# Turning x and z by 32x32 blocks on VectorE, scaling at the output, and turning h inside layer 2, in a kernel of windowed attention, a mixture of experts and a wide second MLP

## The reference

```python
# 1. attention: 2 x 8 heads, 768 positions, head width 64
#    scores against keys nearer than 16 positions and against 24 block summaries; softmax; values
x = attention(q, k, v).transpose(0, 2, 1, 3).reshape(1536, 512)
# 2. mixture of 8 experts, one expert for each token
logits = x @ w_gate + modality_bias[modality_id]          # 1536 x 8
e_idx = argmax(logits); gate_w = softmax(logits)[e_idx]
out[mask] = gate_w[mask, None] * (np.maximum(x[mask] @ w1[e], 0.0) @ w2[e])   # w1: 512 x 1024, w2: 1024 x 512
# 3. second MLP
h = np.maximum(out @ w_in, 0.0)                           # w_in: 512 x 2048
return (h * h) @ w_out                                    # w_out: 2048 x 512
```

## Time and profile before

| | us |
|---|---|
| median of three runs | 522.28 |
| the profiled execution | 521.77 |
| its span, first to last instruction | 520.1 |
| PE busy in the span | 508.1 |
| DVE busy | 225.4 |
| ACT busy | 188.0 |
| granted TensorE clock, mean | 0.998 |

### The profile page before, as it was taken

The page is one execution under the profiler, slowest core; times in us unless marked ns, Lnnn a source line. Parts: engine busy times, 40 slices in busy tenths (PEclk is TensorE's granted clock), DMA queues, the critical chain, the costliest instruction groups (busy, mean ns, idle before and its releaser), DMA issues.

```text
span 520.1 us, 9415 instructions
## 1 busy us (share of the span) xinstructions
PE 508.1 (98%) x3115; PEld 410.0 (79%) x3117; DVE 225.4 (43%) x440; ACT 188.0 (36%) x355; POOL 87.1 (17%) x110
## 2 busy tenths in 40 slices
PE   8889999999999999999999999999999999999995
PEld 3678788888888888888788888888888888888884
DVE  4787686974323554237632422342242233222221
ACT  1876665243524544225522212331221233122121
POOL 4434335027600223100000000300000020000002
PEclk9999999999999999999999999999999999999999
DMA  8999666384661655521200000400000020000002
GB/s 285 336 290 340 235 220 228 99 285 104 189 216 41 219 204 202 202 82 40 83 1 1 0 1 0 161 0 0 0 0 0 0 81 0 0 0 0 0 0 81
DMA packets 19018, 54.92 MB, mean 106 GB/s; under 512 B 2848, under 2 KB 3120, under 8 KB 18480
## 3 DMA queue, kind: packets, MB, share of 16 engines
q1 hardware_dynamic: 11200, 27.47, 16.6%
q0 software_dynamic: 5200, 23.62, 12.6%
q10 hardware_dynamic: 2592, 3.49, 1.8%
HBM read 42.51 MB, written 12.07 MB: 105 GB/s over the span
## 4 chain that ended last, share of the span: by engine, by line
PE 95%; DVE 3%; issue 1%; ACT 1%; POOL 0%; POOLq 0%; DVEq 0%; ACTq 0%
PE psum L1653 9%; PE psum L1654 9%; PE psum L1652 9%; PE psum L1668 8%; PE psum L1669 8%; PE psum L1670 8%; PE psum L1536 5%; PE psum L1559 5%; PE psum L1538 5%; PE psum L1560 5%; PE psum L1561 5%; PE psum L1537 5%; PE psum L1396 2%; PE psum L1569 2%; PE psum L1371 2%; PE psum L1456 2%
## 5 line engine op out<-in xcount | busy, mean ns | idle before, releaser
L1326 DVE TENSOR_TENSOR sq<-r_sb 128x512 f32<-128x512 f32 x48 | 33.2, 692 | 141.4 <-ACT r_sb L734 137.4
L734 ACT ACTIVATE r_sb<-psum 128x512 f32<-128x512 f32 x48 | 28.7, 597 | 143.7 <-PE psum L1654 143.7
L1668 PE MATMUL psum<-W,s_hi 128*128 128x512 f32 x192 | 75.9, 395 | 0.1
L1653 PE MATMUL psum<-z_lo,W 128*128 128x512 f32 x192 | 75.8, 395 | 0.0
L1654 PE MATMUL psum<-z_hi,W 128*128 128x512 f32 x192 | 75.8, 395 | 0.0
L1652 PE MATMUL psum<-z_hi,W 128*128 128x512 f32 x192 | 75.8, 395 | 0.0
L1669 PE MATMUL psum<-W,s_hi 128*128 128x512 f32 x192 | 75.5, 393 | 0.0
L1670 PE MATMUL psum<-W,s_lo 128*128 128x512 f32 x192 | 75.4, 393 | 0.0
L893 POOL DMA_INDIRECT out<-o_sb,sorted_m x12 | 11.6, 969 | 293.5 <-DVE o_sb L1342 291.6
L1328 DVE TENSOR_TENSOR s_lo<-sq,s_hi 128x512 fp32r<-128x512 f32 x48 | 33.2, 692 | 33.5 <-ACT s_hi L736 33.5
L736 ACT ACTIVATE s_hi<-sq 128x512 fp32r<-128x512 f32 x48 | 30.3, 632 | 41.8 <-DVE sq L1326 41.8
(11 more groups left out here) (205 smaller groups left out, 729.5 us busy)
## 6 DMA issues: line engine op xcount, KB each, us to landing
raw<-in_w POOLq DMA_DIRECT2D x4, 2048.0 KB, 9.1
raw<-in_w_io POOLq DMA_DIRECT2D x4, 2048.0 KB, 8.2
v_in<-in_v SPq DMA_DIRECT2D x12, 390.0 KB, 12.7
raw<-in_w SPq DMA_DIRECT2D x8, 512.0 KB, 4.3
kT<-in_kT SPq DMA_DIRECT2D x8, 400.0 KB, 7.9
q_in<-in_q SPq DMA_DIRECT2D x12, 256.0 KB, 8.8
X<-in_vT SPq DMA_DIRECT2D x4, 768.0 KB, 11.7
x_in<-xs_d SPq DMA_DIRECT2D x12, 256.0 KB, 2.8
```

What stands on the lines that cost most here:

```text
L1326: dve.tensor_tensor(sq[:, :], r_sb[:, :], r_sb[:, :], ALU.mult).then_inc(sem["sqs"], 1)
L1653: pe.matmul(bank[f % 2][:, :], wh, z_lo[:, k, :], start=False, stop=False)
L1668: pe.matmul(bank[2 + j][:, :], s_hi[f % SBUFS][:, tok], wh, start=(f == 0), stop=False)
```

## The change

The columns of x and z are taken in another order, d = 4 p + k for partition p of chunk k, in place of d = 128 k + p; the host lays w1, w2 and w_in out to match. In that order a turn by 32x32 blocks on VectorE is enough, if the load spreads the rows over the partitions by quarters of their columns.

- x of tiles 4 to 12 is loaded with pieces of 512 bytes and turned by one DVE instruction into `x_w`, in the step before the one that splits it; PE no longer turns it. Tiles 0 to 3 stay on PE, and their transposes now read every fourth column.
- z is loaded by four transfers of 32 partitions each, and each of its four chunks is turned by one DVE instruction into `z_w`, which lies where `z_lo` lies. The first group is loaded once the loads of x are all issued, and turned at the end of step 11. No z is turned on PE, and none is scaled. g^2 is computed once (`g_sq`) after the loop and applied in the copies of the finished rows; ACT waits for it before its part of the second MLP.
- `h_transpose(t)` runs inside `layer2(t - 1)`, ahead of its last six matmuls, and reads every fourth column. In the loop, ACT's high part of h now also waits for the half (`l2m`) and the end (`l2`) of `layer2(t - 1)`. y has two PSUM banks, and DVE copies it after the low part of h, not ahead of it.
- `layer2(12)` is issued inside the loop, right behind `layer2(11)`.

```diff
@@ sync @@
             def load_x(t, s):
                 row = sp.value_load(table[0:1, bass.ds(t + T_ROW, 1)], min_val=0, max_val=E * EROWS)
-                sp.dma_start(x_in[s][:, :], xs_d[bass.ds(row, P), :]).then_inc(s_xs[s], 16)
+                if isinstance(t, int) and t <= SPEC:
+                    sp.dma_start(x_in[s][:, :], xs_d[bass.ds(row, P), :]).then_inc(s_xs[s], 16)
+                else:
+                    sp.dma_start(x_in[s][:, :], xs_d[bass.ds(row, P), :].rearrange("(a j) (q f) -> q a j f", a=QW, f=P)
+                                 ).then_inc(s_xs[s], 16)
+
+            def load_z(g, into):
+                for q in range(KD):
+                    sp.dma_start(into[q * QW:(q + 1) * QW, :], quarter(ys_d[g * GT * P:(g + 1) * GT * P, :], q)
+                                 ).then_inc(sem["zin"], 16)
@@ scalar, moe_step @@
-                x_high(t + 1)
+                if isinstance(t, int):
+                    x_high(t + 1)
+                else:
+                    with act.If(t < last):
+                        x_high(t + 1)
+                    with act.If(t == last):
+                        parts_high()
                 for h in range(2):
                     act.wait_ge(sem["ht"], t * 2 + (h + 1))
+                    if not isinstance(t, int):
+                        act.wait_ge(sem["l2" if h else "l2m"], t)
@@ scalar, second MLP @@
+            act.wait_ge(sem["gsq"], 1)
             with act.If(swapped == 1):
                 out_second(range(PARTS, 2 * PARTS))
...
-                    act.activation(o_sb[:, j, :], bank[2 + j][:, :], ACT.Copy).then_inc(sem["o_a"], 1)
+                    act.activation(o_sb[:, j, :], bank[2 + j][:, :], ACT.Copy, scale=g_sq[:, bass.ds(g * GT + j, 1)]
+                                   ).then_inc(sem["o_a"], 1)
@@ vector @@
+            def x_turn(t, s, lapx):
+                dve.wait_ge(s_xs[s], lapx * 16)
+                dve.wait_ge(sem["x_l"], t)
+                dve.transpose(turned(x_w[:, :, :]), blocks(x_in[s][:, :])).then_inc(sem["x_t"], 1)
...
+            def loop_step(t, s, lap):
+                with dve.If(t < last):
+                    x_low(t + 1, True)
+                with dve.If(t == last):
+                    z_low(0)
+                h_low(t)
+                dve.wait_ge(s_ys[s], lap * 16 + 16)
+                y_copy(t - 1, y_sb[s], s)
+                with dve.If(t + 1 < last):
+                    x_turn(t + 2, 1 - s, lap + 1 + s)
+                with dve.If(t == last):
+                    out_low(range(PARTS))
+                    y_copy(last, y_last, 1 - s)
+                low_next(t - 1, range(PARTS, PARTS + 2))
+                low_next(t, range(PARTS))
+                with dve.If(t + 1 == last):
+                    parts_turn()
...
+            def z_turn(z, k):
+                dve.transpose(z_w[:, k, :].rearrange("p (a j) -> p j a", a=QW), blocks(z[:, :])[:, :, k, :]
+                              ).then_inc(sem["zt"], 1)
...
+            x_turn(SPEC + 1, 0, 2)
             with dve.Fori(0, (TILES - SPEC) // 2) as m:
...
+            dve.wait_ge(sem["sorted"], 16)
+            dve.tensor_tensor(g_sq[:, :], sorted_m[:, 0:NB, 0], sorted_m[:, 0:NB, 0], ALU.mult).then_inc(sem["gsq"], 1)
...
                 with dve.If(g < GROUPS - 1):
-                    z_low(g + 1)
+                    dve.wait_ge(sem["zin"], (g + 2) * (KD * 16))
+                    dve.wait_ge(sem["m1"], g * KFF + KFF)
+                    z_turn(z_in, 0)
+                    for k in range(KD):
+                        if k + 1 < KD:
+                            z_turn(z_in, k + 1)
+                        z_low(g + 1, (k,))
@@ tensor @@
             def h_transpose(t):
                 for h in range(2):
                     pe.wait_ge(sem["relu"], t * 2 + (h + 1))
                     for k in range(4):
-                        c = (4 * h + k) * P
-                        ins = pe.transpose(bank[2 + h][:, k * P:(k + 1) * P], h_of(t)[0][:, c:c + P], ident[:, :])
+                        half = h_of(t)[0][:, h * DM:(h + 1) * DM].rearrange("p (f k) -> p k f", k=KD)
+                        ins = pe.transpose(bank[2 + h][:, k * P:(k + 1) * P], half[:, k, :], ident[:, :])
...
                 layer1(t, *weights_of(t), between=((KD // 2, lambda: last.extend(weights_of(t - 1))),))
-                x_transpose(t + 1, s, lapx)
-                layer2(t - 1, *last)
-                h_transpose(t)
+                layer2(t - 1, s, *last, between=((KF - 2, lambda: h_transpose(t)),))
...
-                        moe_step(t + 1, 1, m + 2)
+                        moe_step(t + 1, 1)
+                        with pe.If(t + 2 == n_t):
+                            layer2(t + 1, 0, swapped, n_run)
+                    with pe.If(t + 1 == n_t):
+                        layer2(t, 1, swapped, n_run)
...
-            part_transposes()
-            layer2(n_t - 1, swapped, n_run)
```

More of the change, by code:

```diff
@@ L291, in build @@
     cursor["c"] = after_moe
-    z_part = [sb("c", f"z_part{s}", [P, DM], F32) for s in range(2)] + x_in
+    x_w = sb("c", "x_w", [P, KD, P], F32)
+    z_q = nc.alloc_sbuf_tensor_at("z_q", [P, GT * DM], F32, offset=cursor["c"])
     z_hi = sb("c", "z_hi", [P, KD, GT * P], F32R)
+    z_w = nc.alloc_sbuf_tensor_at("z_w", [P, KD, GT * P], F32, offset=cursor["c"])
     z_lo = sb("c", "z_lo", [P, KD, GT * P], F32R)
+    g_sq = sb("c", "g_sq", [P, NB], F32)
     psum = nc.alloc_psum_tensor("psum", [P, 8, 512], F32)
@@ L330, in build @@
         meta metas sorted rows placed slots rout oh tab n_run e0 x0 warm early lsub scat_b scat_c scat_d x2
-        raw0 raw1 zfill scat_a x_t x_h x_l l1 relu ht hh hl l2 y sh sla slbv slbp
-        counts both ylast wo_h wo_v zin scale zt zh zl m1 r sqs s_h s_l mo o_a o_v out ofree den_ok""".split()
+        raw0 raw1 zfill scat_a x_t x_h x_l l1 relu ht hh hl l2 l2m y sh sla slbv slbp
+        counts both ylast wo_h wo_v zin gsq zt zh zl m1 r sqs s_h s_l mo o_a o_v out ofree den_ok""".split()
     sem = {n: nc.alloc_semaphore("s_" + n) for n in names}
@@ L402, in x_bank, with y_bank, quarter, turned @@
         return bank[3] if isinstance(t, int) and t == 0 else bank[5]
[L404 to L410, removed]
+    def y_bank(s):
+        return bank[7 if s else 4]
+    def quarter(ap, q):
+        return ap[:, q * P:(q + 1) * P]
+    def turned(ap):
+        return ap.rearrange("p k (a j) -> p j k a", a=QW)
+    def blocks(ap):
+        return ap.rearrange("p (j c k) -> p j k c", c=QW, k=KD)
     block = nc.Block()
@@ L508, in _ @@
                 t = m * 2 + SPEC
-                with sp.If(t + 1 < n_t):
+                with sp.If(t + 2 < n_t):
                     moe_step(t + 1, 0)
-                    with sp.If(t + 2 < n_t):
+                    with sp.If(t + 3 < n_t):
                         moe_step(t + 2, 1)
[L513 to L522, removed]
+            load_parts()
             at = sp.value_load(table[0:1, bass.ds(n_t - 1 + T_POS, 1)], min_val=0, max_val=N)
@@ L660, in parts_high @@
             def parts_high():
[L661 to L664, removed]
+                act.wait_ge(sem["zt"], KD)
+                for k in range(KD):
+                    act.activation(z_hi[:, k, :], z_w[:, k, :], ACT.Copy).then_inc(sem["zh"], 1)
             def moe_step(t, s=None, before=None):
@@ L1207, in moe_step @@
             def moe_step(t, s, lap):
[L1208 to L1212, removed]
                 if isinstance(t, int) and t == 1:
@@ L1543, in layer1, with layer2 @@
                         do()
-            def layer2(t, slot, run, between=()):
-                halves = isinstance(t, int)
-                pe.wait_ge(sem["hl"], t * 2 + 1 if halves else t * 2 + 2)
-                pe.wait_ge(sem["y"], t + AHEAD)
+            def layer2(t, s, slot, run, between=()):
+                pe.wait_ge(sem["hl"], t * 2 + 1)
+                if not isinstance(t, int) or t > 1 - AHEAD:
+                    pe.wait_ge(sem["y"], t - 1 + AHEAD)
                 for k in range(KF):
@@ L1552, in layer2 @@
                             do()
-                    if halves and k == KF // 2:
+                    if k == KF // 2:
                         pe.wait_ge(sem["hl"], t * 2 + 2)
@@ L1589, in _ @@
             layer1(1, 0, 1)
-            layer2(0, 0, 1, between=((6, lambda: x_transpose(2, 0, 1)),))
+            layer2(0, 0, 0, 1, between=((6, lambda: x_transpose(2, 0, 1)),))
             h_transpose(1)
@@ L1599, in _ @@
             layer1(2, 0, 1, between=((2, load_counts),))
-            layer2(1, 0, 1, between=((6, lambda: x_transpose(3, 1, 1)),))
+            layer2(1, 1, 0, 1, between=((6, lambda: x_transpose(3, 1, 1)),))
             pe.wait_ge(sem["both"], 1)
```

129 lines of the change are left out of this document (55 added, 74 removed).

## The result

The changed kernel took 516.45 us, the median of 16 runs (514.43 to 519.68), beside 522.44 for the kernel before (16 runs, 520.22 to 526.58). The ratio is 0.9888, 95% interval [0.9863, 0.9912]: 6.0 us less by the medians, where 6.0 less was forecast. The profiled execution took 518.67 us (span 517.0, mean granted clock 0.995). It is 2.2 us above the median. So the comparison starts at that turn. From it to the first `down` of the second MLP is 139.43 us (before 141.0), from there to the end of the span 265.04 (268.81): -1.57 and -3.77, together -5.3 us.

The account below looks back on a forecast made before the run. PE was taken to bound the kernel, busy 508.1 of 520.1 us. The terms -3.96 + 1.4 + 0.4 + 0.1 - 3.9 = -6.0 us, from the profiled 521.77, gave 515.8 us, range 511.5 to 524.

Parts of the forecast that it names:

- the likeliest case: The forecast itself for the whole kernel: 513.5 to 518 us; chance 0.45.
- x leaves PE: Ten groups of four transposes of x leave PE; nine stand ahead of layer1(12), 0.44 us each: -3.96 us.
- the groups: Between the second MLP's later groups, PE's 10.20 us lose the 1.95 beyond its matmuls: -3.9 us for two.
- The price of a stride: PE's 120 transposes that read every fourth column: taken at nothing, upper bound +0.11 us each or +13 us.
- Rival 1: PE's strided transposes run at half speed: 120 x 0.11 = +13, 529 us; chance 0.18.
- DVE's turn: Turning 128x512 on DVE instead of PE: taken as 0.7 us, at the far end 1.4 us.
- Step of tile 4: Loop step of tile 4: late weights on ACT make relu late for PE's turn of h, delaying layer1(5): +1.4 us.
- The heavy steps: Steps of tiles 7 and 9: relu has no margin for PE's turn of h inside layer2; 0.2 us each, +0.4.
- Start of the second MLP: From layer1(12) to the first `down`: 2.8 us gained are given back as PE waits for g_sq and relu, +0.1 us.

## Why the prediction was right, and what was off

The time, the sign and the likeliest case were right, and so was the mechanism in its main: transposes leave PE, and late waits give a part back. Several terms were off, by 0.3 to 1.3 us and with both signs. That the medians give the 6.0 us of the sum to the digit is luck.

- **x leaves PE** (-3.96) and **the groups** (-3.9): the second measured -3.94. For the first, nine steps at 11.96 in place of 12.34 us make -3.42; 11.90 was forecast, and without the stride it is 11.86 to 11.88.
- **The price of a stride**, taken at nothing between 0 and 0.11 us a transpose, is 0.011: 0.09 us a step, 0.8 in nine steps, and an estimated 1.3 for all 120 transposes (those of x were not tested). Of all terms this one was mis-sized by most. The sentence on the cacheline in the Trainium skill (SBUF — State Buffer, "Door 1: The DMA port swizzle") held in direction, for PE's weight load (141 to 208 ns) and DVE's turn (0.70 to 1.1 us) alike. Rival 1 fell because only 11 of the 67 ns show in the pace of the transposes.
- **DVE's turn** at 0.7 is right for the operation (0.70 without strides) and wrong for its operands: 1.12. PE's stretch between groups is 8.23 us all the same, since the fourth chunk was done at 9.5 us, not at the 8.5 forecast, and PE wants it at 10.4.
- **Step of tile 4**, +1.4: +0.91, and by another path. The weights started 2.3 us behind the store, not 4.2, relu was in time for the turn, and PE stood behind the turn for "issue". What failed here was to take the 4.22 us of one profile as a fixed distance.
- **The heavy steps**, +0.4: 0.73 in three steps, those of tiles 7, 8 and 10, where tiles 7 and 9 were named. In the step of tile 7 the times behind the start of layer1 were right to 0.1 us (store 2.4, relu 8.9, PE at 9.6). But the mechanism was another: relu was in time for its turn, and the gap came behind it, ahead of layer1. The two larger gaps stand in steps that were said to have 0.6 us more room; behind both the loop jumps back.
- Up to layer1(12) this makes 110.84 us behind h of tile 2, before 112.14: -1.30, where -2.16 was forecast.
- **Start of the second MLP**: the first `down` 28.59 us behind layer1(12), forecast 29.0. The exit of DVE, g_sq, then ACT's relu came in that order. PE's wait was foreseen as 3.2 us in one place; it was 1.33 and 0.92 in two, the first of them PE's own exit, which the sum had left out. g_sq came 2.5 us behind the copy, not 3.9: the rest of the 3.9 lies behind the place of g_sq.

To the first `down` -1.57 us came of -2.06, behind it -3.77 of -3.9: 5.3 us by one profiled execution of each kernel, 6.0 by the medians. The two differ by 0.7 us, less than the interval of the ratio, which is 2.6 us wide.

## What to carry to other kernels

A loop with a fixed bound and a test inside makes its unused passes free only as long as some engine has work behind them. Before you shorten the work behind a loop, look for the "issue" there, and count it as the next thing that is late: here it gave back 2.25 of some 8 us. A bound that fits these inputs won it back in the profile. The two forms that hold for every input (a bound from a register, two levels) did shorten the exit, but their ratios are 0.9953 and 0.9954, beside 0.9888 for the changed kernel: here they lost more than they won.

When an operation moves to another engine, price it with its operands' strides: a plain copy's row gives the lower end, and a stride here added 60% to DVE's turn and 10% to PE's transposes.

## What the runs showed of the hardware

- A turn of 128x512 float32 by 32x32 blocks on DVE: 0.70 us plain, 1.05 to 1.12 with a stride of 16 bytes on the read, of 64 bytes on the write, or with both.
- DVE's subtraction of two operands in SBUF waits for a subtraction of GpSimd that is under way, at times for the next one too: 0.69 us alone, 1.16 to 5.26 beside it, 0.89 to 1.37 with the latter in quarters.
- An unused pass of a loop with one test: about 0.7 us on DVE.
- In profiles of kernels with small edits the steps of tiles 4 and 5 together took 24.3 to 33.8 us, the long ones with ACT and PE both standing for "issue". Whether the edit or the execution makes it is open.
- TensorE's granted clock fell from 1.00 to 0.50 (1.2 of 2.4 GHz) for about 3 us, behind two gaps of PE of 1.73 and 0.93 us; a matmul then started each 0.43 us.
